# A decay-attention tree walked level by level over three chunks at once, its score products placed in quadrants of the array

## The reference

```
# attention: B=4, H=8, S=768, D=48; f = sigmoid(f_logit)
state[t] = f[t] * state[t-1] + outer(k[t], v[t])        # D x D per head; f scales the rows
y[t]     = q[t] @ state[t]
# MLP on x = y, its heads side by side (384 wide):
x = x + relu(layernorm(x) * g @ w1) @ w2                # w1 384 x 1536, w2 1536 x 384
# gated convolution:
h = relu(x @ w3); c = conv(h, 3 taps along the sequence) # w3 384 x 1024
out = (h * sigmoid(c)) @ w4                             # w4 1024 x 384
```

## Time and profile before

| | |
|---|---|
| median of 3 runs | 852.27 us (851.37 to 854.04) |
| the profiled execution: its own time | 854.34 us |
| its span in the profile | 852.6 us |
| PE busy | 783.9 us (92% of the span), 5200 records |
| PEld busy | 753.9 us (88%) |
| DVE busy | 624.2 us (73%), 1425 instructions |
| ACT busy | 419.1 us (49%) |
| POOL busy | 190.9 us (22%) |
| score products, L770 | 170.3 us, 1152 records |
| phase B begins | at 642.8 us |

### The profile page before, as it was taken

How to read it: one execution, slowest core, us unless ns; L and a number is a source line. 1 busy time by engine, 2 the same in 40 slices (tenths; PEclk the granted TensorE clock), 3 DMA queues, 4 the chain that set the end, 5 groups by cost and what they waited for, 6 DMA issues and landing times. The chain is left out here.

```text
span 852.6 us, 15035 instructions
## 1 busy us (share of the span) xinstructions
PE 783.9 (92%) x5200; PEld 753.9 (88%) x5200; DVE 624.2 (73%) x1425; ACT 419.1 (49%) x900; POOL 190.9 (22%) x203
## 2 busy tenths in 40 slices
PE   3676899989989998998999899899998999999998
PEld 3566889989978997997899899799997999999997
DVE  6975886796688679658867866975255877777775
ACT  3461454336245333624534453451245767777775
POOL 8573232133124114212411430340000000000000
PEclk9755899999999999999999999999999999999999
DMA  7358321242071134207114320110331011111001
GB/s 212 102 138 217 77 90 48 63 124 93 2 180 53 48 81 105 93 3 186 47 48 99 103 78 29 47 48 1 134 99 56 4 54 57 56 55 55 28 2 55
DMA packets 22072, 65.46 MB, mean 77 GB/s; under 512 B 2384, under 2 KB 14160, under 8 KB 22000
## 3 DMA queue, kind: packets, MB, share of 16 engines
q1 hardware_dynamic: 22000, 64.52, 26.6%
HBM read 55.08 MB, written 9.44 MB: 76 GB/s over the span
## 5 line engine op out<-in xcount | busy, mean ns | idle before, releaser
L770 PEld LDWEIGHTS bank<-QZ,K 128*128 128x128 f32 x1152 | 153.1, 204 | 72.3 <-DVE AT L664 36.1
L770 PE MATMUL bank<-QZ,K 128*128 128x128 f32 x1152 | 170.3, 295 | 50.7 <-ACT QZ L502 47.0
L502 ACT COPY QZ<-QP 64x256 f32<-64x256 f32 x288 | 117.5, 408 | 170.4 <-DVE QP L632 166.4
L734 DVE SCALAR_TENSOR_TENSOR HLO<-bank,HHI 128x384 fp32r<-128x384 f32 x96 | 53.5, 557 | 100.2 <-ACT HHI L557 99.5
L1019 DVE SCALAR_TENSOR_TENSOR TB<-HB,CW,TB 128x384 f32<-128x384 f32 x128 | 79.2, 619 | 45.7 <-ACT TB L983 43.4
L557 ACT ACTIVATE HHI<-bank 128x384 fp32r<-128x384 f32 x96 | 47.1, 491 | 121.6 <-PE bank L842 120.3
L840 PE MATMUL bank<-XH,W1H 128*128 128x384 f32 x288 | 103.4, 359 | 2.6 <-issue 1.7
L840 PE MATMUL bank<-HHI,W2H 128*128 128x384 f32 x288 | 103.0, 358 | 0.0
L842 PE MATMUL bank<-XH,W1L 128*128 128x384 f32 x288 | 97.7, 339 | 0.0
L841 PE MATMUL bank<-XL,W1H 128*128 128x384 f32 x288 | 97.2, 337 | 0.0
L842 PE MATMUL bank<-HHI,W2L 128*128 128x384 f32 x288 | 97.1, 337 | 0.0
(11 more groups left out here) (101 smaller groups left out, 1551.7 us busy)
## 6 DMA issues: line engine op xcount, KB each, us to landing
NEAR<-near SPq DMA_DIRECT2D x24, 960.0 KB, 4.7
XB<-x2d SPq DMA_DIRECT2D x8, 577.5 KB, 4.7
X<-w SPq DMA_DIRECT2D x12, 384.0 KB, 5.5
V<-v SPq DMA_DIRECT2D x8, 576.0 KB, 11.6
x2d<-X SPq DMA_DIRECT2D x8, 576.0 KB, 3.7
F<-f SPq DMA_DIRECT2D x14, 288.0 KB, 5.9
Q<-q SPq DMA_DIRECT2D x14, 288.0 KB, 8.1
K<-k SPq DMA_DIRECT2D x14, 288.0 KB, 10.8
```

The source lines that it names most:

```text
L502: ins = nc.scalar.copy(QZ[rows, c, :, par, :].rearrange("p j (n m) -> p j n m", m=m), one)
L770: ins = mm(sb_[slot % 2][:, j * P:(j + 1) * P], K[u.par][:, c, j, :], QZ[:, c, j].rearrange("p a b -> p (a b)"), start=True, stop=True)
```

## The change

- The tree goes level by level over the whole unit: one `prep` for all three chunks, one `score` step per level, six in place of 18. `base` is made for the whole unit at once (in the first unit in two parts).
- QZ and `scatter` are gone. PE reads K and QP in place: for each chunk, pair, head (its 48 rows) and half of the chunk one product of 64 stationary columns of K and the 32 second-block positions of QP, into `pair`, two banks, one per head. Rows and columns of the array fall into quadrants of 64x64. At the last level, whose blocks are 64, there is one product of 64 by 64 per chunk, pair and head.
- The masked copies are made at levels 0 to 2, four per level of 64 partitions and 384 elements each; ACT copies levels 3 to 5 (four, two and four copies).
- `near(c)` stands at level 2c, `near_y(c)` at level 2c+1, ahead of `lastprep` at the last. Two MLP steps follow each level. In the ends `y`, `kv` and `norm` are one group, and one MLP step follows each of the six groups (ENDS = 6).
- In `y` each product is made in two halves of 64 stationary columns.

```diff
-STAGES = 6
-SLOTS = STAGES * NC
-MASKED = 4 * NC
+QUARTER = 32
+CP = NC * NP
+LEVELS = 6
+MASKED = 3
+PARTS = (slice(0, 1), slice(1, NC))
-NEAR_LAG = 2
-ENDS = 3
+ENDS = 6
...
-        def scores(shift, lag):
-            groups = [[("score", s)] for s in range(SLOTS)]
+        def scores():
+            groups = [[("score", st)] for st in range(LEVELS)]
             for c in range(NC):
-                at = c * SLOTS // NC + shift
-                groups[at].append(("near", c))
-                groups[at + lag].append(("near_y", c))
+                groups[2 * c].append(("near", c))
+                groups[2 * c + 1].append(("near_y", c))
             groups[-1].append(("lastprep", 0))
...
-            ends += [[("ktr", c)] + ([("scale", c - 1)] if c else []), [("y", c)], [("kv", c), ("norm", c)]]
+            ends += [[("ktr", c)] + ([("scale", c - 1)] if c else []), [("y", c), ("kv", c), ("norm", c)]]
...
+            def base(u, _):
+                for i, part in enumerate(PARTS):
+                    whole = part if u.first else slice(0, NC)
...
+                    Kc = K[u.par][:, whole].rearrange("p c j t -> p (c j) t")
+                    Fc = F[u.par][:, whole].rearrange("p c j t -> p (c j) t")
+                    tt(blocks(Kc, 1, 0), blocks(Kc, 1, 0), blocks(Fc, 1, 1), ALU.mult)
+                    tt(QP[:, whole], Q[u.par][:, whole], F[u.par][:, whole], ALU.mult
+                       ).then_inc(base_ready, 1 if u.first else 2)
+                    if not u.first:
+                        return
+            def prep(u, st):
+                Kc, QPc = (a[:].rearrange("p c j t -> p (c j) t") for a in (K[u.par], QP))
                 if st:
-                    dve.wait_ge(score_done, u.count(SLOTS, i - NC + 1))
+                    dve.wait_ge(score_done, u.count(LEVELS, min(st, LEVELS)))
+                    dve.wait_ge(prep_ready, u.count(PREPS, st))
...
+            def score(u, st):
+                if st < MASKED:
+                    dve.wait_ge(score_done, u.count(LEVELS, st + 1))
...
+                    for g in range(2):
...
+                        for par in range(2):
...
+                            ins = nc.vector.copy_predicated(to, mask.broadcast_to([HALF, CP, QUARTER // m, m]), of)
+                    ins.then_inc(mask_done, 1)
+                if st + 1 < LEVELS:
+                    prep(u, st + 1)
...
+            def score(u, st):
+                pe.wait_ge(prep_ready, u.count(PREPS, st + 1))
+                if st > MASKED:
+                    pe.wait_ge(copy_done, u.count(COPIED, st - MASKED))
+                elif st:
+                    pe.wait_ge(mask_done, u.count(MASKED, st))
+                elif not u.first:
+                    pe.wait_ge(xl_ready, u.count(KT, -1))
+                pe.sem_inc(score_go, 1)
+                m = 2 << st
+                for c in range(NC):
+                    for j in range(NP):
+                        for par in range(2):
+                            rows = slice(HALF * par, HALF * par + D)
+                            if m == HALF:
+                                at = (2 * c + j % 2) * HALF
+                                ins = mm(pair[HALF * (j // 2):HALF * (j // 2) + HALF, par, at:at + HALF],
+                                         K[u.par][rows, c, j, 0:HALF], QP[rows, c, j, HALF:], start=True, stop=True)
+                                continue
+                            at = (c * NP + j) * QUARTER
+                            for g in range(2):
+                                half = slice(HALF * g, HALF * g + HALF)
+                                right = QP[rows, c, j, half].rearrange("p (n two m) -> p n two m", two=2, m=m)[:, :, 1, :]
+                                ins = mm(pair[half, par, at:at + QUARTER], K[u.par][rows, c, j, half], right,
+                                         start=True, stop=True)
...
             def ktr(u, c):
-                pe.wait_ge(prep_ready, u.count(PREPS, PREPS - NC + c + 1))
+                pe.wait_ge(prep_ready, u.count(PREPS, PREPS))
...
                     for h in (2 * j, 2 * j + 1):
-                        ins = mm(yb[:, D * h:D * h + D], AT[:, c, h, :], V[u.par][:, c, D * h:D * h + D],
-                                 start=first, stop=True, skip_group_check=True)
+                        for half in (slice(0, HALF), slice(HALF, C)):
+                            ins = mm(yb[half, D * h:D * h + D], AT[:, c, h, half], V[u.par][:, c, D * h:D * h + D],
+                                     start=first, stop=True, skip_group_check=True)
```

More of the change, by code:

```diff
@@ L282, in phase_a @@
             up_down += [("up", g), ("down", g - 1)]
-        FIRST = ([("gates", 0), ("base", 0), ("open", 0)] + merge(scores(1, 3), [("weights", i) for i in range(NW1)])
+        FIRST = ([("gates", 0), ("base", 0), ("open", 0)] + merge(scores(), [("weights", i) for i in range(NW1)])
                  + merge(ends, [("weights", i) for i in range(NW1, NW)])
@@ L423, in _ @@
                                          pattern=[[-1, P]], channel_multiplier=1))
-            for st in range(MASKED // NC):
+            for st in range(MASKED):
                 m = 2 << st
@@ L490, in _ @@
             act.sem_inc(x2_ready, KT)
[L492 to L503, removed]
-            def gates(u, _):
[L506 to L519, removed]
+            def gates(u, _):
+                for part in PARTS:
+                    if u.first and part.start == 0:
+                        act.wait_ge(f_ahead, 32)
+                    else:
+                        act.wait_ge(f_in[u.par], u.nth(32, 32))
+                    nc.scalar.activation(F[u.par][:, part], F[u.par][:, part], ACT.Sigmoid).then_inc(f_ready, 1)
             def near_(u, c):
@@ L523, in near_ @@
                 nc.scalar.activation(NEAR[:, NF], NEAR[:, NF], ACT.Sigmoid).then_inc(near_gate, 1)
[L525 to L531, removed]
-                    for n in range(HALF // m):
[L533 to L537, removed]
+            def score(u, st):
+                if st < MASKED:
+                    return
+                act.wait_ge(score_done, u.count(LEVELS, st + 1))
+                m = 2 << st
+                to = AT[:].rearrange("p c (j par) t -> p par (c j) t", par=2)
+                if m == HALF:
+                    to = AT[:].rearrange("p c (jh jl par) t -> p jh par c jl t", par=2, jl=2)
+                    of = pair[:, :, 0:CP * QUARTER].rearrange("p par (c jl t) -> p par c jl t", c=NC, jl=2)
+                    for jh in range(2):
+                        for par in range(2):
+                            ins = nc.scalar.copy(to[0:HALF, jh, par, :, :, HALF:], of[HALF * jh:HALF * jh + HALF, par])
+                else:
+                    of = pair[:, :, 0:CP * QUARTER].rearrange("p par (cj n m) -> p par cj n m", cj=CP, m=m)
+                    for n in range(HALF // m):
+                        at = 2 * m * n
+                        ins = nc.scalar.copy(to[at:at + m, :, :, at + m:at + 2 * m],
+                                             of[at:at + m, :, :, n % (QUARTER // m), :])
+                ins.then_inc(copy_done, 1)
             def ktr(u, c):
@@ L581, in xb @@
                     nc.scalar.copy(nxt.XBH[0][:, d], nxt.XB[0][:, d]).then_inc(nxt.xbh_ready, 1)
[L583 removed]
+            walk(act, dict(wb=wb, xb=xb, gates=gates, near=near_, score=score, ktr=ktr, xnt=xnt, up=up, x2=x2, weights=weights))
         @block.vector
@@ L593, in _ @@
             tt = nc.vector.tensor_tensor
[L595 to L608, removed]
```

100 lines of the change are left out of this document (45 added, 55 removed).

## The result

The changed kernel takes 895.5 us (median of 4 runs, 890.4 to 899.0) against 852.6 us of the kernel before: a ratio of 1.0498, 95% interval 1.0441 to 1.0555. It is slower, as forecast, and 907 was 1.3% too high. Two executions of one experiment (e_quads), 887.2 and 889.7 us, ran at a lower mean clock over the whole program, 0.94 against 0.97, and are left out of the comparison there.

What follows compares the result with a forecast made beforehand. A unit was taken as PE work with small gaps. Slower by 6.6 us per unit, 46 over seven units, plus 9 in the first: +55 on 854.3 gives 909, as a median 907 us; range 840 to 942.

Steps and rivals of the forecast that it cites:

- The serial chain: Score stage: each level's scores wait for DVE's preparation, the last one behind near_y(2); first transpose 6.4 us later per unit.
- The gap of 3.1 us after level 0: Score stage: PE idle for 3.1 us while DVE finishes masked copies and the next preparation.
- The waits before down(5) and before the transpose: End of score stage: down(5) starts at 41.8 instead of 40.6; PE then idle 4.0 us before the first transpose.
- the smaller gaps: Score stage: PE waits 1.3 us each for the preparations ahead of scores 2 and 3.
- The pitch of the quadrants: Score products on PE: 0.031 us per record, bounds 0.016 and 0.053, so a level of 96 records takes 3.2 us.
- rival (a): Score products: four quadrants at once, 0.016 us pitch, chain stays, +23 us, 875 us as a median; chance 0.18.
- the two near links: Near-neighbour chain on DVE, transfer and POOL: 12.3 us from the start of DVE's reduction to the end of POOL's operations.
- Value products: Products of y in halves: 1.75 us per chunk instead of 2.71, 2.8 us less per unit.
- The clock: PE's granted clock falls after the 4.0 us gap before the transposes: 1.6 us lost per unit.
- The base step: One base step for all chunks, 2.5 us on DVE ahead of the last scale: 0.8 us more per unit.
- The first unit: First unit, without blocks beside its scores and mostly at half clock: first transpose at 65.7, +9 us after value products.
- the blocks between the products: Ends of the unit: transposes and products stand apart with blocks between, three more entries and exits, 0.6 us.

Runs made afterwards that it cites:

- e_quads: Kernel before with quadrant products alone, read in place without scatter, still chunk by chunk in 18 slots: 865.4 and 869.0 us.
- e_near2: Changed kernel with two NEAR buffers instead of one: 840.3 us, ratio 0.9836 to the kernel before.
- e_lastprep: Changed kernel with the last preparation ahead of the last near_y: 875.0 us, ratio 1.0252 to the kernel before.
- e_three: Changed kernel with MLP blocks 3, 2, 2, 2, 2, 1 after the six levels: 890.4 us, ratio 1.0436 to the kernel before.
- e_twoquad: Changed kernel with two NEAR buffers and score products ordered with two quadrants in turn: 897.9 us, one run.
- e_halves: Kernel before with only the value products of y made in halves of 64 columns: 832.4 us, ratio 0.9754.
- e_slack: Changed kernel with two NEAR buffers, last preparation ahead of the last near_y, and blocks 3, 2, 2, 2, 2, 1: 826.8 us, ratio 0.9688.
- e_slack13: e_slack with one more MLP block after level 2, taken from the ends (3, 2, 3, 2, 2, 1): 813.4 us, ratio 0.9542.
- e_filler: e_near2 with eight products that nobody reads put after the first up and down block behind level 0: 841.0 us.

## Why the prediction was right, step by step

**The serial chain held.** The gap of 3.1 us after level 0 was forecast and is 3.12. near_y was forecast at 16.9, 30.9 and 43.2 us after the unit's first score and came at 15.0, 28.9 and 42.2; the first transpose at 47.5 and came at 46.0 (44.1 to 46.2 in the six units from 174 us on). The waits before down(5) and before the transpose were 1.2 and 4.0 and are 4.0 and 2.7. A unit was forecast at about 79 us and takes 78.5. e_near2, e_lastprep and e_three show that this chain sets the time: mended, reordered, and left while another gap was filled. Of the smaller gaps, 1.3 us each, the one ahead of level 2 was not there in the unit shown, the one ahead of level 3 was 1.09, and one of 1.39 ahead of level 4 was not forecast.

**The pitch of the quadrants was the step that failed.** I took 0.031 us, "because the two records of one product use the same quadrant and follow each other, as at L813", and kept 0.016 as a bound and as rival (a). Measured: 0.0147. e_twoquad shows where the scaling was sound, 0.027 for two quadrants in turn, and where it stopped. A pair of records comes back to its quadrant after two, four and eight pitches with one, two and four in turn: 0.104, 0.109 and 0.118 us. So a pair occupies its quadrant for about 0.11 us whatever the others do, and what I had scaled as a pitch was this time shared by two; the loop shares it by four. This is worked out from the three pitches; no run shows what in the quadrant takes the time. On this the rule of the Trainium skill, TensorEngine Tiling (Array Packing), section Tiling Modes, that tiles load weights and multiply independently of one another, was right, and the trace agrees: 0.052, 0.027, 0.0147 us for one, two and four. The other rule that I cited from the same page, some 60 cycles for every matmul (Performance Considerations, Instruction Overhead; 25 ns at the full clock), the trace contradicts: 14.7 ns from start to start.

**Why the total was near nonetheless.** In part by luck. Rival (a) had the pitch and gave 875, 20 us too low. It had the three near_y at 14.1, 27.4 and 39.7 and the transpose at 44.0; they came at 15.0, 28.9 and 42.2, and the transpose at 46.0. The first 0.9 us is level 1 at half the clock: in the three units in which it ran at the full clock the first near_y came 13.8 to 13.9 us after the first score. The rest is the two near links, 13.9 and 13.3 us where (a) has 13.3 and 12.3: POOL's operations took 1.55 to 1.71 us beside DVE's longer preparations instead of 1.0, and DVE was not free at once. So the chain took back what the faster products gave, and my two errors, products too slow and links too short, had opposite signs. Five levels quicker by 1.6 us each bought 1.5 us: with the near chain last, PE's products hardly count.

**The other terms.** Value products: 1.75 us per chunk forecast, 1.63 measured; alone 21 us. The clock: 1.6 us per unit forecast for the fall before the transposes. The distance from first to second transpose exceeds that of the same unit in e_near2 by 0 to 2.7 us in the seven units, 1.7 in the mean. The fall after the gap at level 0, which I had left to the range, came in all of the six units from 174 us on. In three it took in level 1 (2.78 or 2.79 us); in the other three level 1 ran at the full clock and the blocks behind it at half:

```profile
426.20:431.00 4.80, 4.80 (x23) 4.63 (x18) 4.63 (x9) 0.49 (x1) 0.00 (x0) 0.64 0.00 0
```

It costs most when it takes in level 1, which is on the chain: the score stages of the first three took 45.7 to 46.2 us, those of the other three 44.1 to 44.9. The base step: 0.8 us forecast, 0.33 us in PE's wait ahead of the last transposes of the result. The first unit: +9 forecast, +4.4 measured; its first transpose is at 63.13 where 65.7 was forecast. The difference arises ahead of the first near_y, which came at 32.0 instead of 34.6: the second level, put at 9.2 us, took 7.3.

**In sum** 6.6 us per unit were forecast and 5.2 measured. The score stage without the three moved blocks grew by 4.1 us in the mean of the seven units (6.4 forecast), what follows it by 1.1 (0.2 forecast). In the second part the halves give 3.0 (e_halves), the clock costs 1.7, the base step 0.3 and the two waits of 3.6 us at first up blocks 0.8 more than such waits before; 1.3 us is left where 0.6 was forecast for the blocks between the products.

## What to carry to other kernels

When a loop over chunks is turned into one step over all of them, ask first what else was timed by the loop: here a single buffer, whose refill has to wait for its last reader (9.35 us from a reduction to POOL's next operation), harmless with near steps spread over 18 slots, set the pace of the six levels. Write down the times of every chain that the new list makes, also of those that the diff does not touch, and mend the one that is last before judging the change. On small products let successive ones go to different quadrants. And ask again after each mend what is last: with the near chain last, levels 1.6 us quicker than forecast brought the end of the score stage 1.5 us forward; with that chain mended, levels 1.2 us longer (e_twoquad) cost 6.5 us per unit.

## What the runs showed that I had not expected

- The four quadrants' pitch above, and that the order of the same products moves a level from 1.60 to 5.16 us.
- Stretches in which PE waits for nothing that the profile shows grew with the number of instructions. In the changed kernel one of 1.31 us stands after the 43rd of a level's 96 records (again at 349.3, 0.28 long), and two of 3.6 us at a first up block, where before PE's longest such wait at an up block was 1.0 us:

```profile
189.00 0.88 PE L770 MATMUL bank<-QP,K 48*64 48x32 f32 x43
191.20 1.01 PE L770 MATMUL bank<-QP,K 48*64 48x32 f32 x53 [1.31 <-issue]
...
412.38 0.34 PE L842 MATMUL bank<-XH,W1H 128*128 128x384 f32 x1 [3.61 <-issue]
```

  The instruction queue brought 1.20 MB in 73 packets instead of 0.70 MB in 43. The other runs show that such a stretch belongs to a place in PE's list of instructions. It stands after the 43rd record of level 2 in the changed kernel, in e_near2 and in e_lastprep; after the 34th in e_three, e_slack and e_slack13, which have one block of nine products more ahead of it; after the 27th in e_filler, which has two fillers of eight ahead of it in each turn of the loop over batches. The stretches of 3.6 us stand where this loop turns.

```profile
193.67 1.54 PE L777 MATMUL bank<-QP,K 48*64 48x32 f32 x62 [2.08 <-issue]
...
180.52 1.24 PE L784 MATMUL bank<-QP,K 48*64 48x32 f32 x69 [0.97 <-issue]
```

  (e_three, then e_filler.) A wait for data would not move with the count of instructions ahead. That PE waits for the instructions themselves fits both places, but no run changed how they are brought, so it is not shown.
- Moving one block to the place of a gap was worth 13 us (e_slack to e_slack13), 1.9 us per unit for a block of 1.57 us, where 1.0 to 1.6 were expected. What gave the rest was not tested.
